# Score matmuls of the later tiles in blocks of 32 key positions, two head pairs interleaved

## The reference, cut to what matters

```python
for t in range(S):
    kt, vt, rt = (k[:, :, t], v[:, :, t], r[:, :, t])
    cur = np.einsum('bhd,bhe->bhde', u[None] * kt, vt)
    y[:, :, t] = np.einsum('bhd,bhde->bhe', rt, state + cur)
    state = w[None, :, :, None] * state + np.einsum('bhd,bhe->bhde', kt, vt)
...
# first layer:  h = x @ w_in;  g = relu(h)**2;      x = g @ w_out
# second layer: h = x @ w_in;  g = h - tanh(h);     out = g @ w_out
```

## Time and profile before

| | |
|---|---|
| Median of 3 runs | 879.99 us (879.98 to 881.31) |
| Profiled execution: time | 880.22 us |
| Profiled execution: span, first to last instruction | 878.2 us |
| Instructions profiled | 15490 |
| PE busy | 865.5 us, 99% of the span |
| DVE, POOL, ACT busy | 597.0, 501.2, 453.5 us |

### The profile page before, as it was taken

The page is one execution under the profiler, slowest core; times in us unless marked ns, Lnnn a source line. Parts: engine busy times, 40 slices in busy tenths (PEclk is TensorE's granted clock), DMA queues, the critical chain, the costliest instruction groups (busy, mean ns, idle before and its releaser), DMA issues.

```text
span 878.2 us, 15490 instructions
## 1 busy us (share of the span) xinstructions
PE 865.5 (99%) x6115; PEld 714.6 (81%) x6115; DVE 597.0 (68%) x812; ACT 453.5 (52%) x859; POOL 501.2 (57%) x378
## 2 busy tenths in 40 slices
PE   8999999999999999999999999999999999999998
PEld 6778888888888888888888788888888888888886
DVE  7887656636654664453465687787787787787775
ACT  7543223222223323221234777777777777777775
POOL 8856645444543534332348676666666666666664
PEclk9999999999999999999999999999999999999999
DMA  7642111303111130202122000000000100100100
GB/s 269 248 133 81 59 60 60 118 1 114 64 59 60 60 115 4 89 30 108 37 72 72 0 1 1 37 1 1 37 1 0 37 1 1 37 0 1 37 1 36
DMA packets 12168, 47.06 MB, mean 54 GB/s; under 512 B 1472, under 2 KB 2112, under 8 KB 12096
## 3 DMA queue, kind: packets, MB, share of 16 engines
q1 hardware_dynamic: 12096, 46.08, 15.0%
HBM read 41.36 MB, written 4.72 MB: 52 GB/s over the span
## 4 chain that ended last, share of the span: by engine, by line
PE 86%; DVE 4%; POOL 4%; DMA 3%; issue 2%; ACT 1%; SPq 0%; ACTq 0%; DVEq 0%; POOLq 0%
PE acc L648 14%; PE acc L650 13%; PE acc L649 13%; PE hid L650 10%; PE hid L648 10%; PE hid L649 10%; PE sc L650 3%; PE sc L648 3%; PE sc L649 3%; DMA x2T<-in_nat 2%; PE y L713 2%; PE y L697 1%; PE sc L682 1%; DVE area L909 1%; POOL wout_l L398 1%
## 5 line engine op out<-in xcount | busy, mean ns | idle before, releaser
L392 POOL TENSOR_TENSOR g_l<-g_f,g_h 128x512 fp32r<-128x512 f32 x96 | 130.9, 1364 | 172.4 <-ACT g_h L493 172.4
L648 PE MATMUL acc<-g_h,wout_h 128*128 128x512 f32 x564 | 222.2, 394 | 0.6 <-POOL g_l L408 0.6
L650 PE MATMUL acc<-g_h,wout_l 128*128 128x512 f32 x564 | 219.7, 389 | 0.0
L649 PE MATMUL acc<-g_l,wout_h 128*128 128x512 f32 x564 | 219.6, 389 | 0.0
L493 ACT ACTIVATE g_h<-g_f 128x512 fp32r<-128x512 f32 x96 | 60.5, 630 | 272.3 <-DVE g_f L948 271.7
L403 POOL TENSOR_TENSOR area<-area 128x512 f32<-128x512 f32 x96 | 125.7, 1310 | 103.9 <-ACT area L511 103.9
L648 PE MATMUL hid<-x_h,win_h 128*128 128x512 f32 (+1 forms) x435 | 169.0, 388 | 0.0
L649 PE MATMUL hid<-x_l,win_h 128*128 128x512 f32 (+1 forms) x435 | 168.6, 388 | 0.0
L650 PE MATMUL hid<-x_h,win_l 128*128 128x512 f32 (+1 forms) x435 | 168.5, 387 | 0.0
L408 POOL TENSOR_TENSOR g_l<-g_f,g_h 128x512 fp32r<-128x512 f32 x96 | 128.6, 1339 | 32.8 <-ACT g_h L526 32.8
L1014 DVE TENSOR_SCALAR area<-area 128x512 f32<-128x512 f32 x96 | 87.2, 909 | 58.8 <-POOL area L403 58.8
(11 more groups left out here) (136 smaller groups left out, 1152.4 us busy)
## 6 DMA issues: line engine op xcount, KB each, us to landing
x2T<-in_nat SPq DMA_DIRECT2D x10, 736.0 KB, 5.8
area<-in_nat SPq DMA_DIRECT2D x10, 736.0 KB, 5.1
x2T<-in_tt SPq DMA_DIRECT2D x10, 512.0 KB, 4.1
area<-in_tt SPq DMA_DIRECT2D x10, 512.0 KB, 3.6
out<-x2T SPq DMA_DIRECT2D x18, 256.0 KB, 2.2
x2T<-in_win SPq DMA_DIRECT2D x4, 768.0 KB, 6.5
x2T<-in_wout SPq DMA_DIRECT2D x4, 768.0 KB, 6.8
area<-in_win SPq DMA_DIRECT2D x4, 768.0 KB, 4.4
```

The source lines that it names most:

```text
L392: pool.tensor_tensor(g_l[:, m % 4, :], g_f[:, m % 2, :], g_h[:, m % 4, :].bitcast(F32), ALU.subtract).then_inc(s_gl1, 1)
L648: pe.matmul(dst, wh, xh, start=first, stop=False)
L649: pe.matmul(dst, wh, xl, start=False, stop=False)
L650: return pe.matmul(dst, wl, xh, start=False, stop=last)
```

## The change

Only `score` is changed. For T = 4 to 23 a matmul now covers 32 key positions (32 columns of the array) in place of 64, so that its moving operand is 128, 96, 64 or 32 columns long, whatever lies behind the block's first key. The first four tiles keep their halves. For all tiles the order within the program is new: two pairs are taken together, and matmuls of the same length stand side by side.

```diff
-                for a in range(PAIRS):
-                    for half in (1, 0):
-                        first = HP * half if a % 2 == 0 else HP - HP * half
+                wide = HP if T < TPB else 32
+                parts = P // wide
+                for even in range(0, PAIRS, 2):
+                    order = []
+                    for q in range(parts // 2):
+                        order += [(even, q), (even + 1, parts - 1 - q)]
+                    for q in range(parts // 2):
+                        order += [(even + 1, q), (even, parts - 1 - q)]
+                    for a, q in order:
+                        first = wide * q if a % 2 == 0 else P - wide - wide * q
+                        ks = slice(wide * q, wide * q + wide)
                         for g in range(2):
                             rows, to = slice(HP * g, HP * g + HP), 512 * g + P * a
-                            mm = pe.matmul(dst[HP * half:HP * half + HP, to + first:to + P],
-                                           kT[rows, a, HP * half:HP * half + HP], rT[rows, a, first:P],
+                            mm = pe.matmul(dst[ks, to + first:to + P], kT[rows, a, ks], rT[rows, a, first:P],
                                            start=True, stop=True)
                 mm.then_inc(s_sc, 1)
```

## The result

| | median | runs | ratio to before, 95% interval |
|---|---|---|---|
| before | 879.99 us | 12 (879.29 to 881.77) | |
| changed | 882.82 us | 12 (881.68 to 886.36) | 1.0033 (1.0025 to 1.0040) |

The forecast was 878.5 us, in a range of 877.8 to 880.3. The time moved the other way, by 2.8 us.

The account below looks back on a forecast made before the run. PE was taken as the bound, 86% of the last-ending chain. 15 steady score groups at 0.10 us save 1.5 us, five early groups and startup nothing: 879.99 to 878.5 us, range 877.8 to 880.3.

Parts of the forecast that it names:

- What bounds the kernel, and who waits for a score: PE leads from 95 us on; DVE's mask waits for 15 score groups (tiles 9 to 23), so only those count.
- Step (1): Score group on eight 32-column blocks takes 0.727 us where it was 0.83, 0.10 us saved.
- Step (2): Twice the matmuls in each score group, 1280 more PE instructions over 20 groups, run in parallel blocks and cost nothing.
- the slow end (0.13): 128 instructions of a score group at 7.5 ns each would take 0.96 us, 0.13 more; 15 groups, 2 us.
- theory A: Recorded before the experiments: PE holds 64 instructions in program order; the 65th enters only when the first has ended.
- Step (4): Attention and next mask move up with the shorter score; masks end 0.05 us before L735, a tie kept without new wait.
- The early slots, at nothing: Slots of tiles 4 to 8: DVE starts the mask no earlier, PE waits out the gain; five groups bring nothing.
- Floor, or blocks in each other's way: Short records have a floor or blocks wait their turn; 0.05 us a group left, 879.3 us; chance 0.12.
- All 20 groups with the gain: Slots of tiles 4 to 8 move up too; 2.0 to 2.2 us gained, 877.9 us; chance 0.12.
- Slower: Eight blocks don't run at once: some 887 us with four, 881.2 with six; slow instruction supply included; chance 0.10.
- The Trainium skill's 60 cycles: Weighed rule: 32-column records would cost 52 and not 29 ns, taking 0.09 of the 0.10 us saved a group.

Follow-up runs that it names:

- e6: Kernel before (64-column halves) with the two mask copies split by PSUM bank instead of by odd and even pairs; 879.48 us, ratio 0.9993.
- e7: Changed kernel with the two mask copies split by PSUM bank instead of by odd and even pairs; 880.96 us, ratio 1.0004.
- e12: Changed kernel with the scores of pairs 2 and 3 left out for tiles 4 to 23; 875.66 us (one measurement).
- e11: Kernel before with the halves' matmuls of pairs 2 and 3 issued twice for tiles 4 to 23; 884.84 us (one measurement).
- e2_short_first: Changed kernel with 32- and 64-column matmuls ahead of 128s and 96s in each two pairs, tiles 4 to 23; 882.84 us, ratio 1.0026.
- e3_best: Changed kernel with a searched order of the quarters over all four pairs, tiles 4 to 23; 881.51 us, ratio 1.0012.
- e10: Changed kernel with quarters, in its order, for tiles 4 to 8 only and halves for all others; 881.06 us, ratio 1.0008.
- e4: Changed kernel with each pair's quarters in plain order 3, 2, 1, 0, tiles 4 to 23; 882.67 us, ratio 1.0024.

## Why the prediction was wrong

**What bounds the kernel, and who waits for a score: right.** PE leads from 95 us on, and each of the 15 steady groups counts: 0.098 us each inside the slot and 0.073 by the start of the next one, once the mask's wait was out of the way (e6, e7). The medians' 1.48 us can't tell 1.1 from 1.5.

**Step (1), the price of the group: wrong, in sign.** I had 0.727 us for it and it took 0.926. The arithmetic of eight blocks was right within 0.02 us: half a group takes 0.437 us (e12), where the same sum gives 0.277 + 0.14 + 0.033 = 0.45, and 32-column records follow each other 29 ns apart in their blocks (the single starts are 0.242 and 0.271 us behind the group's). What failed is the step behind it:

**Step (2), "I cost it at nothing".** I asked whether 128 instructions could be supplied in 0.554 us, at a pace from 33 ns of the trace, and found that they could. That pace (4.2 ns an instruction) was even right. But by theory A the four starts that it came from were out of a queue that had filled during the long matmuls before. What I hadn't asked is how far ahead of the oldest unfinished instruction the queue reaches. The kernel before has 64 instructions in a score group, on four blocks, where even 96 cost nothing (e11), and so never met the limit. The Trainium skill gives it (TensorE: Matmul & The Clock Gate, its table at the head and Part 3): a queue of 64 with a partial reorder window. The changed kernel agrees, with its stop just behind the first 64 instructions (33 records and 34 loads had started at the stop); I had read past it. The outcome, 0.1 us a group slower, is near what I had kept as the slow end (0.13), for another reason; that is luck.

**Step (4), the tie: wrong.** I read the 0.05 us between the masks' end and L735 as a lead. It is the delay after a wait: L735 stands 0.11 us behind L713's last start in the kernel before and 0.09 in e6, so it waited 0.02 us a slot already. And "kept, with no new wait" supposed that the mask starts at a fixed distance behind the last score record. It started 0.07 us behind that record's end in the kernel before, and 0.11 in the changed one, 0.09 in e2_short_first, 0.15 in e3_best. So L735 fell behind the attention by another 0.045 us, in 12 slots 0.5 us. Taking the wait out (e7) gave back 0.92 us of the rest, 785.92 to 785.00, and 1.9 us of the median, more than the steady slots' 0.5: it took out the whole wait, 0.07 us a slot, with the part that the kernel before had too, and a mask copy less counts in the early slots as well.

The two make 12 x 0.14 + 3 x 0.1 = 2.0 us; the rest grew by 1.90 us in the profiles. Of the 2.8 us between the medians some 0.9 are left, for what comes before.

**The early slots, at nothing: wrong, the cause shown in part.** In the changed kernel's profile they are 1.36 us late at 95.6 us, 0.79 of it from the startup, in e10's 0.7 us at 94.9, and e10's median is 0.75 us up, with an interval that just holds zero; e2, e3 and e4 put 1.2 to 1.7 us there. The chain passes through the scores in the slot of tile 6 in the changed kernel, which it did not before:

```profile
77.05 0.93 PE sc L690 x34
77.97 0.79 PE y L704 x24
78.77 0.87 PE y L720 x32
79.64 0.49 PE sc L742 x32
80.14 6.65 DMA x2T<-in_nat
```

So the reading that no early score can count held for one execution of one timing. The step of 0.7 us in the changed kernel and in e10 is DVE's instruction beside POOL's, above; how the quarters bring POOL's start there, and what costs the time in e2 and e4, I haven't shown.

**The rivals.** Floor, or blocks in each other's way: neither, by e12, and by e3, where unlike neighbours are the fastest. All 20 groups with the gain: no gain, so untested as put. Slower: it happened, but not by too few blocks at once; eight ran. The Trainium skill's 60 cycles (TensorEngine Tiling (Array Packing), Instruction Overhead), which I had weighed against the change as 60 columns and so 52 ns: the 32-column records start 29 ns behind each other. The rule itself isn't refuted by it, since 60 cycles at 2.4 GHz would be 25 ns, by an estimate from that page; I had turned cycles into columns.

## What to carry to other kernels

Count instructions, not only time, when a matmul is cut smaller: a 32-bit matmul is four, and with more than 64 in a dense group on eight blocks the order within the group decides (0.76 to 0.93 us for the same work here). By theory A short ones early free the queue, but simply putting them first took 0.878 us, still more than the halves' 0.828; only the searched order was faster. Before a gain on an engine is booked, look for what ends at the same moment as it does: here PE already waited 0.02 us a slot for a DVE copy, and a shorter group gave nothing until that copy was off PE's way. The sign of such a wait was a gap that is the same, 0.05 us, wherever PE is known to wait. A pace taken from a few starts after a long instruction may be that of a full queue, as theory A has it here.

## What the hardware showed that I had not expected

PE starts matmuls of different blocks out of the program's order: in the slot at 214.55 us the ninth matmul of the group (32 columns) started at 214.79 and the thirteenth (64 columns), on another block, at 214.77. And the time from the modelled end of a group's last record to the waiting DVE copy isn't fixed: 0.07 us with four blocks (64 or 96 instructions), 0.09 to 0.15 with eight and 128, 0.18 with eight and 64 (e12). It doesn't follow the number of instructions, and I have no cause for it.
